# Retention layer before two MLPs, one core: chunk loads of 128 partitions and a two-round output

## The chip, the cores and the metric

The kernel runs on one core of one Trainium2 chip. The metric is the device time of the execution in microseconds (us), and the median of the runs is compared. A core has TensorE (PE, with its weight loads shown apart as PEld), VectorE (DVE), ScalarE (ACT), GpSimd (POOL) and SyncE (SP), which here only issues transfers. The engines run their own instruction streams in order and meet at semaphores.

## The reference

What is computed, cut to its core:

```python
# q, k, v: (2, 8, 576, 64)
scores = (q @ k^T) / sqrt(64)                       # per batch and head
ret = scores * where(i >= j, gamma[h] ** (i - j), 0)
attn = ret @ v
x = attn.transpose(0, 2, 1, 3).reshape(1152, 512)
# mixture of 4 experts, all of them for every token
p = domain_probs / (sum(domain_probs) + 1e-9)
for e in range(4):
    out += p[:, e:e+1] * (max(x @ w1[e], 0) @ w2[e])     # w1[e]: 512x1024, w2[e]: 1024x512
h = out @ w_in                                      # 512x2048
return (h * tanh(softplus(h))) @ w_out              # 2048x512
```

## The kernel before

The attention is computed in chunked form. A sequence of 576 tokens is cut into 9 chunks of 64 (`CH`, `CHUNKS`). For chunk t the output is the part inside the chunk (masked scores times v) plus the part of all earlier chunks, which is carried as a 64x64 matrix per head, the state, times q. Decay is applied to v ahead of time (`v_decay` on POOL) and to the rows of the output (`decayed` on DVE). There are two batches, and 64 rows are half of the 128 partitions, so the two batches lie in the two halves: `TOK[b]` is the half in which batch b has its tokens on the partitions, `FEAT[b]` the half in which it has its features.

**The loads.** A chunk of both batches is 1 MB. SP fetches it by `load_chunk(t)` in two transfers of 64 partitions by 8 KB (L403 and L404), into one of 4 slots (three in `qkv`, the fourth in `last_slot`). A slot has 5 columns: batch 0 has its v beside the q of batch 1, and so on, so that the two halves use different columns for the same kind of data, and each half of the transfer fills four of the five. From chunk 2 on SP first waits until chunk t-2 is there, and from chunk 4 on it also waits for the output of chunk t-4, which frees the slot. Before chunks 4 to 8 it issues two loads of 256 KB each for the MLP weights (`load_weights`, L413), of 128 partitions.

**A turn.** The program runs through `for t in range(CHUNKS)` on each engine. I call round t of it turn t.
PE does in turn t:
- scores of chunk t+1 and the state update of chunk t, interleaved (`scores_and_state`, L441 and L445, 64x64 matmuls). It waits for chunk t+1 to have landed, for the copy of the last state and for `v_decay(t)`.
- `output(t)` (L476): since state and v lie above each other in one column, and q and the masked scores in another, a single matmul of 128 rows does both terms at once. The first chunk has no state and goes by `first_output`, one batch after the other. Two PSUM banks take turns (`ps_o[t % 2]`).
- one or two of the eight first-layer tiles of the first token block (`plain_tile`, 12 matmuls each), placed by the tables `AHEAD` (before the output) and `BEHIND` (after it).

ACT copies the state out of PSUM in two halves (`state_copy`, L697), makes the rounded high part of the weights that have come (`job_hi`, L366) and of x (`first_hi`, L703), and applies relu to finished tiles (`plain_hi`, L714). DVE masks the scores, one instruction of 64 partitions for each batch (`masked`, L815), which writes them over q's place in the slot; it multiplies the output by its decay (`decayed`, L832, one instruction), makes row factors (`rows`, L823) and the low parts (`first_lo` L839, `plain_lo` L845). POOL decays v, one instruction of 64 partitions for each batch (L1026), and makes the low part of the weights (`job_lo`, L393).

**Weights.** All matmuls of the MLPs are done three times, as high by high, high by low and low by high part (L505 to L507). The table `IN_TURN` says in which turn which weight unit is split: "w1" and "w2" are units of the two layers, "s" is a job that forms sums of weight blocks (L380 to L388), since the later stages save multiplications by such sums. `FREE_UNITS` = 3 says how many units of w2 lie in memory that no chunk slot uses; the others wait until the chunks are through. The order on POOL at the end of the attention is unit 3 of w2, then the sums, then units 4 and 5.

After turn 8 PE does 36 matmuls of the second layer (`second(0, q)`, q 0 to 11, three units of tokens for each of the weight units 0 to 3), and then stage 2: `product` P1, two `second(1, q)`, P2, two more `second(1, q)`, then P6, which is the first to need the weight sums. `second(1, 0)` needs unit 4 of w2, `second(1, 3)` unit 5. `keep_warm` issues matmuls of zeros that only keep PE busy.

## Time and profile before

| | us |
|---|---|
| Median of 3 runs | 654.37 (653.7 to 657.46) |
| Profiled execution, its own time | 653.94 |
| Its span in the trace | 652.1 |
| Mean granted TensorE clock of that span | 0.975 |

| Engine | busy us | share of the span |
|---|---|---|
| PE (matmul) | 621.4 | 95% |
| PEld (weight load) | 554.8 | 85% |
| POOL | 288.7 | 44% |
| DVE | 244.4 | 37% |
| ACT | 235.1 | 36% |

Busy time is the union of an engine's instructions. Of the chain of work that ended last PE has 84% and transfers 9%. The trace gives every time from the span's start. PE's busy share by fortieths of the span (16.3 us each) is 60 to 90% in the first six and 90% or more in nearly all others, so what isn't PE at work lies in the first 96 us.

### The profile page before, as it was taken

How to read it: one execution, taken by the hardware profiler on the slowest of the kernel's cores; microseconds unless marked ns; L12 is line 12 of the kernel's file. 1: busy time of each engine (PE TensorE's matmuls, PEld its weight loads, DVE VectorE, ACT ScalarE, POOL GpSimd, SP SyncE). 2: the span in 40 equal slices, each digit the busy share in tenths (PEclk: the TensorE clock that was granted, in tenths of full speed). 3: DMA queues.
4: the chain of work that ended last, by engine and by line, in shares of the span. 5: the costliest groups of instructions: out<-in, count | busy, mean ns of one | idle time of the engine just before them, and what ended most of it. 6: DMA issues, size and time to landing. Idle time of an engine off the chain costs nothing.

```text
span 652.1 us, 9388 instructions
## 1 busy us (share of the span) xinstructions
PE 621.4 (95%) x3768; PEld 554.8 (85%) x3768; DVE 244.4 (37%) x370; ACT 235.1 (36%) x434; POOL 288.7 (44%) x239
## 2 busy tenths in 40 slices
PE   6677969999999999999999999999999999999997
PEld 3566859999999999989999989998979999989996
DVE  2457464333314333314333214334584333314324
ACT  1344242343223333222343223334554554334331
POOL 2356494554343554433544443542363544343300
PEclk8679889999999999999999999999999999999999
DMA  8998231232211133211233201231211233201004
GB/s 194 237 219 194 70 98 46 64 98 81 64 49 33 65 98 98 63 35 33 64 103 92 65 33 33 66 112 66 64 49 33 65 98 83 63 17 25 1 1 121
DMA packets 24170, 50.45 MB, mean 77 GB/s; under 512 B 3008, under 2 KB 3392, under 8 KB 22976
## 3 DMA queue, kind: packets, MB, share of 16 engines
q1 hardware_dynamic: 23152, 48.51, 27.8%
q10 hardware_dynamic: 976, 1.35, 0.8%
q8 instruction: 30, 0.49, 0.3%
q14 instruction: 12, 0.10, 0.1%
HBM read 47.49 MB, written 2.36 MB: 76 GB/s over the span
## 4 chain that ended last, share of the span: by engine, by line
PE 84%; DMA 9%; DVE 2%; POOL 2%; issue 1%; ACT 1%; SPq 1%; POOLq 0%
PE bank L506 28%; PE bank L507 28%; PE bank L505 28%; DMA qkv<-in_chunks 9%; POOL w_lo L393 1%; DVE xt L922 1%; PE bank L628 1%; SPq L403 0%; POOL ws L388 0%; SPq L413 0%; DVE acc_sb L892 0%; DVE acc_sb L896 0%; DVE h_lo L852 0%; DVE acc_sb L1004 0%; POOL ws_f L381 0%
## 5 line engine op out<-in xcount | busy, mean ns | idle before, releaser
L393 POOL TENSOR_TENSOR w_lo<-w_raw,w_hi 128x512 fp32r<-128x512 f32 x96 | 131.7, 1388 | 144.0 <-ACT w_hi L366 143.6
L505 PE MATMUL bank<-w_hi,h_hi 128*128 128x512 f32 x432 | 169.6, 393 | 5.0 <-POOL w_lo L393 5.0
L507 PE MATMUL bank<-w_hi,h_lo 128*128 128x512 f32 x432 | 170.3, 394 | 0.0
L506 PE MATMUL bank<-w_lo,h_hi 128*128 128x512 f32 x432 | 170.0, 394 | 0.0
L388 POOL TENSOR_TENSOR ws<-ws_f,ws 128x1024 fp32r<-128x1024 f32 x24 | 57.8, 2409 | 151.0 <-ACT ws L362 151.0
L879 DVE TENSOR_TENSOR h_act<-part,bank 128x384 f32<-128x384 f32 x96 | 52.9, 551 | 179.8 <-PE bank L507 179.8
L507 PEld LDWEIGHTS bank<-w_hi,h_lo 128*128 128x128 f32 x432 | 81.3, 188 | 17.6
L505 PEld LDWEIGHTS bank<-w_hi,h_hi 128*128 128x128 f32 x432 | 81.3, 188 | 14.9 <-POOL w_lo L393 5.3
L506 PEld LDWEIGHTS bank<-w_lo,h_hi 128*128 128x128 f32 x432 | 81.3, 188 | 9.8
L723 ACT ACTIVATE h_hi<-h_act 128x384 fp32r<-128x384 f32 x64 | 33.6, 526 | 108.1 <-DVE h_act L879 108.1
L505 PE MATMUL bank<-xa_hi,w_hi 128*128 128x384 f32 x192 | 67.2, 350 | 4.6 <-POOL w_lo L393 2.7
L507 PE MATMUL bank<-xa_hi,w_lo 128*128 128x384 f32 x192 | 66.2, 345 | 0.0
L506 PE MATMUL bank<-xa_lo,w_hi 128*128 128x384 f32 x192 | 66.0, 344 | 0.0
L733 ACT ACTIVATE part<-bank 128x384 f32<-128x384 f32 x72 | 35.2, 489 | 83.0 <-PE bank L507 82.2
L845 DVE SCALAR_TENSOR_TENSOR h_lo<-h_act,h_hi 128x384 fp32r<-128x384 f32 x64 | 46.1, 720 | 35.5 <-ACT h_hi L723 35.5
L852 DVE TENSOR_TENSOR h_lo<-h_act,h_hi 128x384 fp32r<-128x384 f32 x48 | 32.8, 683 | 69.2 <-ACT h_hi L728 69.1
L366 ACT ACTIVATE w_hi<-w_raw 128x512 fp32r<-128x512 f32 x96 | 56.8, 618 | 0.0
L505 PE MATMUL bank<-xt,ws 128*128 128x384 f32 x144 | 48.6, 338 | 1.2 <-DVE xt L922 1.2
L506 PE MATMUL bank<-xt,ws 128*128 128x384 f32 x144 | 48.6, 337 | 0.0
L507 PE MATMUL bank<-xt,ws 128*128 128x384 f32 x144 | 48.5, 337 | 0.0
L845 DVE SCALAR_TENSOR_TENSOR h_lo<-bank,h_hi 128x384 fp32r<-128x384 f32 x32 | 17.8, 557 | 81.3 <-ACT h_hi L714 81.3
L714 ACT ACTIVATE h_hi<-bank 128x384 fp32r<-128x384 f32 x32 | 15.7, 492 | 82.1 <-PE bank L507 82.1
(95 smaller groups left out, 895.8 us busy)
## 6 DMA issues: line engine op xcount, KB each, us to landing
w_raw<-in_weights SPq DMA_DIRECT2D x144, 256.0 KB, 2.8
qkv<-in_chunks SPq DMA_DIRECT2D x14, 512.0 KB, 10.1
last_slot<-in_chunks SPq DMA_DIRECT2D x4, 512.0 KB, 10.2
out<-acc_sb SPq DMA_DIRECT2D x6, 128.0 KB, 2.4
out<-acc_sb ACTq DMA_DIRECT2D x6, 128.0 KB, 2.9
out<-acc_sb SPq DMA_DIRECT2D x1, 384.0 KB, 3.9
out<-acc_sb ACTq DMA_DIRECT2D x1, 384.0 KB, 3.8
consts<-in_consts ACTq DMA_DIRECT2D x1, 146.0 KB, 5.1
```

Source lines behind the costliest of these rows:

```text
L366: act.activation(w_hi[:, int(kind == "w2"), x], w_raw[:, r % RAW], ACT.Copy).then_inc(s_wh, 1)
L388: pool.tensor_tensor(w_sum(x)[:, 1], ws_f[:, :], w_sum(x)[:, 0].bitcast(F32), ALU.subtract)\
L393: pool.tensor_tensor(w_lo[:, layer, x], w_raw[:, r % RAW], w_hi[:, layer, x].bitcast(F32), ALU.subtract).then_inc(s_wl, 1)
L505: pe.matmul(out, w[0], x[0], start=first, stop=False, **more)
L506: pe.matmul(out, w[0], x[1], start=False, stop=False, **more)
L507: return pe.matmul(out, w[1], x[0], start=False, stop=last, **more)
L714: act.activation(h_hi[:, tile_slot(s, i)], banks[6 + i % 2][:, 0:TC], ACT.Relu).then_inc(s_hh, 1)
L723: act.activation(h_hi[:, tile_slot(s, i)], h_act[:, i % 2], ACT.Relu).then_inc(s_hh, 1)
L733: act.activation(part[:, i], banks[6][:, 0:TC], ACT.Copy).then_inc(s_pt, 1)
L845: dve.scalar_tensor_tensor(h_lo[:, slot], full, 0.0, h_hi[:, slot].bitcast(F32), ALU.max, ALU.subtract).then_inc(s_hl, 1)
L852: dve.tensor_tensor(h_lo[:, slot], h_act[:, i % 2], h_hi[:, slot].bitcast(F32), ALU.subtract)\
L879: dve.tensor_tensor(h_act[:, i % 2], part[:, kept], banks[bank][:, 0:TC], op).then_inc(s_cc, 1)
```

## The change

It touches only the attention phase and the order of a few weight jobs around it.

- **Layout.** A slot has four columns of 128 partitions, one for each kind: v, k by tokens, k by features, q (`V, KTOK, KF, Q`). In each half stands the batch that belongs there. All four slots lie in `qkv`. A chunk is loaded by one transfer of 128 partitions by 8 KB.
- **Output in two rounds.** `output_of_state(t)` multiplies the state, which ACT now copies over the column KF, by q, 16 matmuls of 64x64; `output(t)` adds masked scores times v, again 16 of 64x64, onto the same PSUM. Each batch has one PSUM bank for all chunks, so the first round of chunk t waits for both `decayed` instructions of chunk t-1 (`s_xt`). Before, the banks alternated by chunk.
- **Masked scores** go to a tensor of their own (`masked_s`, two buffers) by one instruction of 128 partitions. `v_decay` is one instruction of 128 partitions too. `decayed` is two, one for each batch.
- **Weight order.** `FREE_UNITS` is 6. `EARLY_LOADS` puts 1, 2, 2, 2, 2, 2 and 1 weight loads behind (no longer before) the chunks 2 to 8. Unit 4 of w2 is split ahead of the sums, unit 5 after them. Tile 0 moves from behind the output of turn 3 to ahead of it, tiles 2 and 5 to behind the outputs of turns 4 and 6.
- **keep_warm** grows from 11 to 18 matmuls after the first 9.

```diff
-Y1, X0, X1, Z, Y0 = range(5)
-X, Y = (X0, X1), (Y0, Y1)
+V, KTOK, KF, Q = range(4)
...
-FREE_UNITS = 3
+FREE_UNITS = UNITS - 2
...
-AHEAD = {4: 1, 5: 2, 6: 4, 7: 5, 8: 7}
-BEHIND = {3: 0, 5: 3, 7: 6}
+AHEAD = {3: 0, 4: 1, 5: 3, 6: 4, 7: 6, 8: 7}
+BEHIND = {4: 2, 6: 5}
...
+EARLY_LOADS = ((0,), (1, 2), (3, 4), (5, 6), (7, 8), (9, 10), (11,))
...
-    for u in range(3):
-        add(IN_TURN, 6 + (u + 1) // 2, "w2", 0, u)
-    add(IN_TURN, 8, "w2", 0, 3)
-    add(IN_TURN, 8, "s", 0, 0)
-    for u in range(4, 6):
-        add(IN_TURN, 8, "w2", 0, u)
+    for u in range(5):
+        add(IN_TURN, 6 + (u + 2) // 3, "w2", 0, u)
+    add(IN_TURN, CHUNKS, "s", 0, 0)
+    add(IN_TURN, CHUNKS, "w2", 0, 5)
...
-                sp.dma_start(slot(t)[UPPER, 0:4], chunks_in[t, UPPER]).then_inc(s_slot[t % SLOTS], 16)
-                sp.dma_start(slot(t)[LOWER, 1:5], chunks_in[t, LOWER]).then_inc(s_slot[t % SLOTS], 16)
+                sp.dma_start(qkv[:, t % SLOTS], chunks_in[t]).then_inc(s_slot[t % SLOTS], 16)
...
-            for t in range(2, SLOTS):
+            for t in range(2, CHUNKS):
                 chunk_there(t - 2)
                 load_chunk(t)
-            for t in range(SLOTS, CHUNKS):
-                chunk_there(t - 2)
-                for r in range(2 * (t - SLOTS), 2 * (t - SLOTS) + 2):
+                for r in EARLY_LOADS[t - 2]:
                     load_weights(r)
-                load_chunk(t)
...
+            def output_of_state(t):
+
+                pe.wait_ge(s_st, BATCH * t)
+                pe.wait_ge(s_xt, BATCH * t)
+                for h in range(HEADS):
+                    x = h % 2
+                    for b in range(BATCH):
+                        mm = pe.matmul(ps_o[b][DH * x:DH * (x + 1), h // 2], part_of(t, FEAT[b], KF)[:, h],
+                                       part_of(t, FEAT[b], Q)[:, h], start=(h < 2), stop=False, skip_group_check=True)
+                mm.then_inc(s_qs, 1)
 
             def output(t):
 
-                pe.wait_ge(s_vd, BATCH * (t + 1))
-                pe.wait_ge(s_sm, BATCH * (t + 1))
-                pe.wait_ge(s_st, BATCH * t)
-                if t >= 2:
-                    pe.wait_ge(s_xt, t - 1)
-                for hp in range(PAIRS):
+                pe.wait_ge(s_vd, t + 1)
+                pe.wait_ge(s_sm, t + 1)
+                if t > 0:
+                    pe.wait_ge(s_qs, t)
+                for h in range(HEADS):
+                    x = h % 2
                     for b in range(BATCH):
-                        for x in range(2):
-                            mm = output_head(t, b, 2 * hp + x, slice(0, P))
+                        mm = pe.matmul(ps_o[b][DH * x:DH * (x + 1), h // 2], part_of(t, TOK[b], V)[:, h],
+                                       masked_s[TOK[b], t % 2, h], start=(t == 0 and h < 2), stop=True,
+                                       skip_group_check=True)
                 mm.then_inc(s_o, 1)
...
+                if t < PER_BLOCK:
+                    keep_warm(2)
+                if t > 0:
+                    output_of_state(t)
                 if t in AHEAD:
                     plain_tile(AHEAD[t])
-                if t == 0:
-                    keep_warm(3)
-                    first_output()
-                else:
-                    output(t)
+                output(t)
                 if t in BEHIND:
                     plain_tile(BEHIND[t])
+                if t < PER_BLOCK:
+                    keep_warm(2)
...
-                for b in range(BATCH):
-                    dve.tensor_tensor(part_of(t, TOK[b], Y[b]), ps_s[t % 2][FEAT[b]],
-                                      mask[FEAT[b]].unsqueeze(1).broadcast_to([CH, HEADS, CH]), ALU.mult).then_inc(s_sm, 1)
+                dve.tensor_tensor(masked_s[:, t % 2], ps_s[t % 2], mask.unsqueeze(1).broadcast_to([P, HEADS, CH]),
+                                  ALU.mult).then_inc(s_sm, 1)
...
-                dve.tensor_tensor(to.rearrange("p h (b c) -> p h b c", b=BATCH), ps_o[t % 2],
-                                  by.unsqueeze(2).broadcast_to([P, PAIRS, BATCH, CH]), ALU.mult).then_inc(s_xt, 1)
+                for b in range(BATCH):
+                    dve.tensor_tensor(to[:, :, CH * b:CH * (b + 1)], ps_o[b], by, ALU.mult).then_inc(s_xt, 1)
```

On SP, from chunk 2's load to chunk 5's (chunks are counted from 0). In this piece `qkv` and `last_slot` are the chunk slots, `w_raw` the weight ring. Before:

```order
L403 DMA qkv<-in_chunks 64x2048
L404 DMA qkv<-in_chunks 64x2048
L403 DMA last_slot<-in_chunks 64x2048
L404 DMA last_slot<-in_chunks 64x2048
L413 DMA w_raw<-in_weights 128x512 x2
L403 DMA qkv<-in_chunks 64x2048
L404 DMA qkv<-in_chunks 64x2048
L413 DMA w_raw<-in_weights 128x512 x2
L403 DMA qkv<-in_chunks 64x2048
L404 DMA qkv<-in_chunks 64x2048
```

After:

```order
L398 DMA qkv<-in_chunks 128x2048 x2
L407 DMA w_raw<-in_weights 128x512
L398 DMA qkv<-in_chunks 128x2048
L407 DMA w_raw<-in_weights 128x512 x2
L398 DMA qkv<-in_chunks 128x2048
L407 DMA w_raw<-in_weights 128x512 x2
L398 DMA qkv<-in_chunks 128x2048
```

Each chunk is one instruction in place of two, and the weights start earlier: chunk 4's load, the third row that is a chunk load in the piece after, has three weight loads ahead of it where it had two.

On POOL, from the last v decay to the weight sums (`qkv` is v being decayed, `w_lo` the split of a unit, `ws_f` and `ws` the sums). Before:

```order
L1026 TENSOR_TENSOR qkv<-qkv,consts 64x512 x2
L393 TENSOR_TENSOR w_lo<-w_raw,w_hi 128x512 x5
L380 TENSOR_TENSOR ws_f<-w_raw 128x256
L381 TENSOR_TENSOR ws_f<-w_raw 128x256
L383 TENSOR_TENSOR ws_f<-ws_f,w_raw 128x256
L385 TENSOR_TENSOR ws_f<-w_raw,ws_f 128x256
L388 TENSOR_TENSOR ws<-ws_f,ws 128x1024
L393 TENSOR_TENSOR w_lo<-w_raw,w_hi 128x512 x4
```

After:

```order
L1009 TENSOR_TENSOR qkv<-qkv,consts 128x512
L388 TENSOR_TENSOR w_lo<-w_raw,w_hi 128x512 x6
L375 TENSOR_TENSOR ws_f<-w_raw 128x256
L376 TENSOR_TENSOR ws_f<-w_raw 128x256
L378 TENSOR_TENSOR ws_f<-ws_f,w_raw 128x256
L380 TENSOR_TENSOR ws_f<-w_raw,ws_f 128x256
L383 TENSOR_TENSOR ws<-ws_f,ws 128x1024
L388 TENSOR_TENSOR w_lo<-w_raw,w_hi 128x512 x3
```

One more unit of w2 is split ahead of the sums, and one fewer behind them.

## Rows read from the trace of the kernel before

**Rows 1.** Chain of waits, 0 to 62 us: start us, us, what
```profile
1.39 7.45 DMA qkv<-in_chunks
...
32.91 13.64 DMA qkv<-in_chunks
...
47.94 13.73 DMA qkv<-in_chunks
```

**Rows 2.** Busy time by stretch: stretch, its length, engines, granted clock, DMA share, GB/s
```profile
14.00:18.86 4.86, 3.21 (x99) 2.32 (x99) 2.07 (x3) 1.81 (x3) 2.08 (x2) 1.00 1.02 216
31.54:38.76 7.22, 6.04 (x108) 5.42 (x108) 3.40 (x5) 3.35 (x6) 3.35 (x3) 0.76 1.04 228
...
23.00:24.50 1.50, 1.38 (x23) 1.19 (x23) 0.05 (x2) 0.00 (x0) 0.00 (x0) 0.50 1.14 365
29.50:31.00 1.50, 0.00 (x0) 0.00 (x0) 0.69 (x1) 0.63 (x1) 0.00 (x0) 1.00 1.13 350
...
96.00:652.00 556.00, 550.52 (x2761) 496.28 (x2759) 193.95 (x305) 202.33 (x378) 237.53 (x196) 1.00 0.21 61
```

**Rows 3.** Timeline of PE, turns 0 to 5: start, us, instruction [idle before <-releaser]
```profile
15.87 1.43 PE L476 MATMUL bank<-qkv 64*64 64x64 f32 x32
...
31.57 0.27 PE L441 MATMUL bank<-qkv 64*64 64x64 f32 x2 [2.94 <-DMA qkv<-in_chunks]
...
42.36 0.44 PE L505 MATMUL bank<-xa_hi,w_hi 128*128 128x384 f32 x1 [2.41 <-POOL w_lo L393]
...
46.15 1.16 PE L476 MATMUL bank<-qkv 128*64 128x64 f32 x32
47.24 0.27 PE L441 MATMUL bank<-qkv 64*64 64x64 f32 x2
...
48.33 0.44 PE L505 MATMUL bank<-xa_hi,w_hi 128*128 128x384 f32 x1
...
50.62 1.15 PE L476 MATMUL bank<-qkv 128*64 128x64 f32 x32
51.70 0.44 PE L505 MATMUL bank<-xa_hi,w_hi 128*128 128x384 f32 x1
```

**Rows 4.** Timeline of PE, turn 7 to stage 2
```profile
64.82 0.66 PE L505 MATMUL bank<-xa_hi,w_hi 128*128 128x384 f32 x1 [1.94 <-issue]
...
76.00 0.50 PE L505 MATMUL bank<-w_hi,h_hi 128*128 128x512 f32 x1
...
84.29 0.33 PE L505 MATMUL bank<-xb_hi,w_hi 128*128 128x384 f32 x1
...
90.47 0.71 PE L505 MATMUL bank<-w_hi,h_hi 128*128 128x512 f32 x1 [4.95 <-POOL w_lo L393]
...
95.96 0.34 PE L505 MATMUL bank<-xt,ws 128*128 128x384 f32 x1
```

**Rows 5.** Timeline of POOL, 38 to 97 us
```profile
38.81 2.15 POOL L1026 TENSOR_TENSOR qkv<-qkv,consts 64x512 f32<-64x512 f32 x2 [3.65 <-DMA qkv<-in_chunks]
...
56.48 2.53 POOL L393 TENSOR_TENSOR w_lo<-w_raw,w_hi 128x512 fp32r<-128x512 f32 x2
...
79.76 1.46 POOL L380 TENSOR_TENSOR ws_f<-w_raw 128x256 f32<-128x256 f32 x1
...
86.11 2.36 POOL L388 TENSOR_TENSOR ws<-ws_f,ws 128x1024 fp32r<-128x1024 f32 x1 [1.23 <-ACT ws L362]
88.43 7.86 POOL L393 TENSOR_TENSOR w_lo<-w_raw,w_hi 128x512 fp32r<-128x512 f32 x4
```

**Rows 6.** Timeline of ACT, turn 5
```profile
50.73 0.49 ACT L714 ACTIVATE h_hi<-bank 128x384 fp32r<-128x384 f32 x1 [0.70 <-PE bank L507]
51.11 1.14 ACT L366 ACTIVATE w_hi<-w_raw 128x512 fp32r<-128x512 f32 x2
```

**Rows 7.** Timeline of DVE, 52 to 60 us
```profile
52.04 0.55 DVE L845 SCALAR_TENSOR_TENSOR h_lo<-bank,h_hi 128x384 fp32r<-128x384 f32 x1
...
59.49 0.41 DVE L823 TENSOR_TENSOR part<-consts 128x256 f32<-128x256 f32 x1
```

More of the change, by code:

```diff
@@ L183, in build @@
         sb("w_ahead", [P, UNITS + FREE_UNITS, DM], stack=ahead)
-        last_slot = sb("last_slot", [P, 5, HEADS, CH], stack=ahead)
+        masked_s = sb("masked_s", [P, 2, HEADS, CH], stack=ahead)
         ahead.close()
@@ L241, in build @@
         ps_state = banks[2][:, :].rearrange("p (h c) -> p h c", h=HEADS)
-        ps_o = [banks[3 + i][:, :].rearrange("p (h b c) -> p h b c", h=PAIRS, b=BATCH) for i in range(2)]
+        ps_o = [banks[3 + b][:, 0:PAIRS * CH].rearrange("p (h c) -> p h c", h=PAIRS) for b in range(BATCH)]
         s_slot = [sem(f"s_slot{i}") for i in range(SLOTS)]
@@ L440, in scores_head @@
             def scores_head(t, b, h):
-                return pe.matmul(ps_s[t % 2][FEAT[b], h], part_of(t, FEAT[b], X[b])[:, h],
-                                 part_of(t, FEAT[b], Y[b])[:, h], start=True, stop=True)
+                return pe.matmul(ps_s[t % 2][TOK[b], h], part_of(t, FEAT[b], KF)[:, h], part_of(t, FEAT[b], Q)[:, h],
+                                 start=True, stop=True)
             def state_head(t, b, h):
-                return pe.matmul(ps_state[FEAT[b], h], part_of(t, TOK[b], Z)[:, h], part_of(t, TOK[b], X[b])[:, h],
+                return pe.matmul(ps_state[TOK[b], h], part_of(t, TOK[b], KTOK)[:, h], part_of(t, TOK[b], V)[:, h],
                                  start=(t == 0 and h == 0), stop=True, skip_group_check=True)
@@ L639, in _ @@
             scores(0)
-            keep_warm(8)
+            keep_warm(6)
             for t in range(CHUNKS):
@@ L696, in state_copy @@
                 for b in range(BATCH):
[L697 removed]
+                    act.activation(part_of(t + 1, FEAT[b], KF), ps_state[TOK[b]], ACT.Copy).then_inc(s_st, 1)
             def first_hi(t):
[L701 removed]
+                act.wait_ge(s_xt, BATCH * (t + 1))
                 full, hi, lo = x_chunk(t)
@@ L753, in _ @@
                     plain_hi(*divmod(AHEAD[t], ITEMS))
-                if t + 1 < CHUNKS:
-                    for job in IN_TURN.get(t, ()):
-                        job_hi(act, job)
+                for job in IN_TURN.get(t, ()):
+                    job_hi(act, job)
                 first_hi(t)
@@ L759, in _ @@
                     plain_hi(*divmod(BEHIND[t], ITEMS))
-            for job in IN_TURN[CHUNKS - 1]:
+            for job in IN_TURN[CHUNKS]:
                 job_hi(act, job)
@@ L813, in masked @@
                 dve.wait_ge(s_sc, t + 1)
-                for b in range(BATCH):
-                    dve.tensor_tensor(part_of(t, TOK[b], Y[b]), ps_s[t % 2][FEAT[b]],
-                                      mask[FEAT[b]].unsqueeze(1).broadcast_to([CH, HEADS, CH]), ALU.mult).then_inc(s_sm, 1)
+                dve.tensor_tensor(masked_s[:, t % 2], ps_s[t % 2], mask.unsqueeze(1).broadcast_to([P, HEADS, CH]),
+                                  ALU.mult).then_inc(s_sm, 1)
             def rows(i):
@@ L1074, in chunks @@
         vt, kt, kf, qf = by_tokens(v), by_tokens(k), by_features(k), by_features(q)
-        upper = np.stack([qf[1], vt[0], kf[1], kt[0]], axis=2)
-        lower = np.stack([kf[0], vt[1], kt[1], qf[0]], axis=2)
+        upper = np.stack([vt[0], kt[0], kf[1], qf[1]], axis=2)
+        lower = np.stack([vt[1], kt[1], kf[0], qf[0]], axis=2)
         return np.concatenate([upper, lower], axis=1)
```

47 lines of the change are left out of this document (13 added, 34 removed).

## The prediction

> **What bounds the kernel now.** I read the page's busy shares first: PE works through nearly all of the span after the first 96 us, 550.5 of 556 us busy at full clock [rows 2]. Nothing in the change touches that part, so I cost only the stretch up to PE's first matmul with weight sums (P6), which starts at 95.96 us [rows 4], and carry the rest over. Within the stretch I read the chain of waits next. Its long pieces are chunk transfers: 7.45 us for the first, over 13 us for the later ones [rows 1]. Then the windows: while chunks move, the DMA share is 1.02 to 1.04 and the rate 216 to 228 GB/s [rows 2]. The transfers never pause and set the pace, and PE waits for each chunk, 2.94 us for chunk 4 at 31.57 [rows 3]. The last chunk lands at 47.94 + 13.73 = 61.7 us [rows 1]. After it PE has its own backlog, reaches the second layer at 76.00, and then sits 4.95 us at 90.47 for a `w_lo` that stands behind the weight sums on POOL [rows 4, 5]. So there are two things to win: the transfer rate, and that wait.
>
> **The rate.** A chunk is 1.05 MB, and at 216 GB/s it takes 4.9 us. There are two windows in which two weight loads of 128 partitions go through between the chunk halves, and the same queue then moves 365 and 350 GB/s [rows 2], at a DMA share only a tenth higher. The engines are as busy in both, so a load of 64 partitions uses them at lower yield. A chunk loaded on 128 partitions has the weights' shape with longer rows, so I take the lower of the two, 350. The bounds are 216 (nothing gained) and 365.
>
> The Trainium skill ("SBUF — State Buffer", section on the DMA port swizzle) says the same of the halves: partitions 0 to 63 reach only 8 of 16 ports, and 1 MiB moved at 196 GB/s there against 328 on 128 partitions. This case's trace has 216 and 350. By 328 the chunk time below would be 3.2 us in place of 3.0, and the end 1.2 us later.
>
> **When chunk 4 is there.** The first chunk lands at 8.84 [rows 1]; 4.9 of that is transfer, so 3.9 is issue and completion, which stay. Ahead of the end of chunk 4 stand five chunks (5.24 MB), three weight loads (0.79) and some 0.23 MB of constants: 6.26 MB, 17.9 us at 350. Chunk 4 lands at 21.8, against 31.5. Up to there PE has no say: a turn without tiles is one scores round of 1.1 us (47.24 to 48.33 [rows 3]), two output rounds and four `keep_warm`, about 3 us, as long as one chunk.
>
> **PE from turn 3 to the second layer.** From turn 3 on, chunk and weights together need 1.57 MB, 4.5 us each, and PE needs as much or more, so PE takes over. Its work: five scores-and-state rounds of 1.1; eight tiles of 2.3 (48.33 to 50.62 [rows 3]); and six outputs. An output was 1.1 us (50.62 to 51.70 [rows 3]) for 32 records of 128 rows. Now it is 64 records of 64 rows. Two rows bound this: the scores-and-state round does 64 such records in 1.1 us, with four quarters of the array in turn, while `first_output` needed 1.43 us for 32 [rows 3], with consecutive matmuls in the same rows of the array. The new rounds alternate the two batches and so the row halves, like the first, so I take 1.1, no change. Sum: 5.5 + 18.4 + 6.6 = 30.5 us.
>
> The Trainium skill ("TensorE: Matmul & The Clock Gate", Part 3, "The mechanism") speaks against splitting a matmul of 128 rows in two unless they overlap, and lets a weight load overlap a running matmul only where the row group differs. The code alternates them, and the rows above agree. Were they not to overlap, it is the second rival below.
>
> **New stalls, worked out from rows.**
> - Turn 3: tile 0 now stands ahead of the output and needs its `w_lo`. POOL must first decay v of chunk 4: 2.15 us for two instructions of 64 partitions before [rows 5], one now, 1.1 to 1.3 since the same columns pass once. With a `w_lo` of 1.27 (2.53 for two [rows 5]) that is 2.5 us after landing. PE's scores and state output cover 1.7. Stall 0.8.
> - Turn 4: `job_hi` for tile 1 stands on ACT behind tile 0's relu: 0.5 + 0.6 [rows 6], then 1.3 on POOL, with hand-overs 2.9 us from tile to tile. PE has 2.2 us of rounds. Stall 0.6.
> - The added wait: `output_of_state(t)` waits for `decayed(t-1)`, and behind it on PE are the tile and the output, on which in turn all engines wait. `decayed` runs behind `plain_lo` on DVE. After a tile: relu 0.5 [rows 6], low part 0.55, two `decayed` of 0.4 (a 128x256 took 0.41) [rows 7] and hand-overs give 2.1 us, against 1.65 of output and scores round on PE. Some 0.2 to 0.4 in turns 4 and 6; nothing in 5 and 7, behind a second tile; in turn 8, where there is no scores round to cover it, 1.7. Together 2.3.
>
> The masking becomes one instruction in place of two, which helps DVE but isn't on this path. T, the start of the second layer, is 21.8 + 30.5 + 0.8 + 0.6 + 2.3 = 56.0.
>
> **Clock and gaps.** The trace of before is no clean sum either. After PE's 2.94 and 2.41 us waits the granted clock fell to 0.50, which is the 1.2 GHz level, and a tile took 3.8 us (42.36 to 46.15 [rows 3]) in place of 2.3; and there was a 1.94 us gap that nothing in the profile explains [rows 4]. I allow one such tile (1.5) and one such gap (1.9): T = 59.4, against 76.00. That saves 16.6 us. The `keep_warm` added in turns 0 to 2 lies in time that belongs to the transfers; if these are faster than 350, it costs up to 7 x 0.23 us (a matmul of 512 columns, a third of a `second` in the tail below).
>
> **The tail.** From 76.00 to 95.96 are 20.0 us [rows 4]. 4.95 is the wait. The stretch from 90.47 took 5.5 for four `second` of 0.69 ((84.29 - 76.00)/12 [rows 4]) and one product of 1.1, that is 3.8 of work; 1.7 was low clock after the wait. Now unit 4 is split ahead of the sums. Unit 5 is needed at T + 8.3 + 1.1 + 1.4 + 1.1 + 0.7 = T + 12.6. On POOL: unit 4 done at T + 2.1 (relu, `job_hi`, `w_lo` after the last tile, which ends 0.6 before T); the sums took 8.7 us from the first at 79.76 to the end of `ws` at 88.47, ACT's copy among it [rows 5], and give T + 10.8; unit 5 takes 1.3 to 2.0 (7.86/4 [rows 5]) and is there at T + 12.2 to 12.8. So the wait shrinks to 0 to 0.5; I take 0.5. Saved: 4.95 + 1.7 - 0.5 = 6.1.
>
> **Sum.** 16.6 + 6.1 = 22.7 us. The profiled execution took 653.94 by its own time, 0.4 below the median of the runs; 653.94 - 22.7 = 631.2. **I predict 631.**
>
> **Rivals.**
> - The rate stays near 216, because the engines and not the partitions limit it (for: share 1.02 at 216; against: 350 at 1.13). Ahead of chunk 8's end are 12.5 MB: 58 + 3.9 = 62 us. Then a scores round, two tiles, two outputs and the stall of turn 8 are 9.5, T = 71.5, and with the low clock of such a pace 73 to 74. With the tail 2 to 3 + 6.1 saved: 645. Chance 0.10.
> - The rate comes, but the 64x64 rounds don't overlap. Twelve rounds of 1.4 in place of 0.55 from turn 3: +10, 641. Chance 0.12.
> - Slower: the PE of the new turns, with short waits in each, never leaves the 1.2 GHz level from turn 3 to P6. Tiles show the price, 3.8 against 2.3, a factor of 1.65. On 30.5 + 13.3 us of work that is +28.5, less the 1.5 allowed: 658. It decides only if the low level holds in all six turns and the second layer; before, waits of 2 to 3 us brought it on, and it went back each time while PE worked. Chance 0.04.
> - The change doesn't do what it says: chunk 8's load stands on SP behind weight loads that wait for `w_lo` of units 1 and 2 and for the output of turn 4. Both come at about 29 to 31 us, chunk 8 lands by 40, and PE wants it at 45. There are 5 us of cover, so this costs nothing unless turn 4 is 5 us late; then each further us is one us. It is in the range, with no chance of its own.
>
> **How the numbers follow.** Forecast 0.74, rivals 0.10, 0.12, 0.04. The forecast's own range: without allowance for clock and gaps and without the turn 8 stall 626, with the rate of 365 and shorter hand-overs 623; with two more low-clock tiles or a second gap 635. The range takes in the second rival: 622 to 642. What a measurement of this kernel can tell from no change is about 0.5%, 3.3 us. Faster by more than that: the forecast, the first two rivals, less what I may have overlooked in each: 0.92. Same 0.03, slower 0.05.
>
> **What would show it.** Chunk loads land at about 5 us in place of 10; window rates of 330 or more between chunks; chunk 4's scores at 22 us; tiles ahead of outputs at 2.3 us with the clock at 1.00; each output round at 0.6; second layer at 56 to 60; no wait over 1 us before P6; P6 at 73. Wrong would be: rates of 220 (first rival), output rounds of 1.4 (second), clock 0.50 past 35 us (third), PE waiting for chunk 8 (fourth), or any change in the 556 us after P6, which I hold fixed.

## The result, and the profile after

The changed kernel takes 636.98 us (median of 4 runs, 635.42 to 638.36) beside 654.04 for the kernel before in the same set (652.5 to 657.46): a ratio of 0.973, with a 95% interval of 0.968 to 0.978. That is 17.1 us less; I had said 631, 6 us below what came. Two later sets of runs gave 634.3 and 634.65 for the same kernel (ratios 0.974 and 0.972), so 17 to 18 us is its gain. The profiled execution took 638.36, with a span of 636.58, 15.6 less than before (652.14).

From the page of the changed kernel come its busy times, the rates in GB/s by fortieths of the span (15.9 us each), and the group of chunk loads (KB each, us from issue to landing):

```profile
PE 617.0 (97%) x4031; PEld 548.8 (86%) x4031; DVE 238.1 (37%) x370; ACT 234.9 (37%) x434; POOL 278.9 (44%) x230
...
GB/s 344 285 205 116 85 50 66 96 71 66 67 33 67 92 75 67 67 33 67 84 82 67 67 33 68 82 84 34 67 33 34 67 114 84 67 0 26 2 0 124
...
qkv<-in_chunks SPq DMA_DIRECT2D x9, 1024.0 KB, 5.7
```

The chain of waits and the windows answer [rows 1] and [rows 2] (columns as there):

```profile
0.74 5.47 DMA qkv<-in_chunks
```

```profile
6.20:9.30 3.10, 3.04 (x35) 2.22 (x36) 2.59 (x7) 0.00 (x0) 1.04 (x1) 1.00 1.03 433
9.30:12.80 3.50, 3.50 (x103) 2.06 (x102) 2.72 (x5) 1.11 (x2) 2.00 (x2) 1.00 1.02 417
12.80:18.80 6.00, 3.71 (x133) 2.49 (x132) 1.98 (x4) 1.89 (x4) 1.59 (x2) 1.00 0.99 389
...
81.10:636.00 554.90, 549.82 (x2748) 495.59 (x2748) 193.76 (x305) 201.68 (x376) 235.67 (x193) 1.00 0.20 61
```

One chunk transfer is left in the chain where there were many. The DMA share is still about 1, but it now stands for 389 to 433 GB/s instead of 216 to 228. PE's busy share of the long part at the end is what it was.

The timeline of PE through turns 1 to 4 answers [rows 3] (L472 is the new `output_of_state`, L485 the new `output`, L432 and L436 scores and state, L492 the first of a product's three matmuls):

```profile
17.23 0.58 PE L472 MATMUL bank<-qkv 64*64 64x64 f32 x24 [2.11 <-issue]
17.99 0.69 PE L485 MATMUL bank<-masked_s,qkv 64*64 64x64 f32 x32 [0.18 <-PE bank L472]
...
21.96 0.69 PE L472 MATMUL bank<-qkv 64*64 64x64 f32 x30 [0.86 <-issue]
...
23.98 0.27 PE L432 MATMUL bank<-qkv 64*64 64x64 f32 x2
...
27.16 0.27 PE L436 MATMUL bank<-qkv 64*64 64x64 f32 x2 [2.02 <-issue]
...
27.91 0.45 PE L492 MATMUL bank<-xa_hi,w_hi 128*128 128x384 f32 x1
...
30.22 0.69 PE L485 MATMUL bank<-masked_s,qkv 64*64 64x64 f32 x32
...
33.68 0.37 PE L432 MATMUL bank<-qkv 64*64 64x64 f32 x2 [2.07 <-issue]
```

After the first chunk no wait of PE in this execution names a transfer. What is left is four gaps with no releaser (the rows say `<-issue`), 7.06 us together (before: 3.93 us in three). Both output rounds last 0.6 to 0.7, and the first tile 2.3.

The turns' end and the tail, which answer [rows 4]: the wait of turn 8, the start of the second layer (T), P6, and P7, the product behind P6.

```profile
58.74 0.69 PE L472 MATMUL bank<-qkv 64*64 64x64 f32 x32 [1.30 <-DVE xf L820]
...
62.28 0.50 PE L492 MATMUL bank<-w_hi,h_hi 128*128 128x512 f32 x1
...
75.77 0.34 PE L492 MATMUL bank<-xt,ws 128*128 128x384 f32 x1
...
81.10 0.44 PE L492 MATMUL bank<-xt,ws 128*128 128x384 f32 x1 [2.73 <-ACT part L723]
```

The 4.95 us wait for `w_lo` is gone, and a wait of 2.73 stands in a place that had none. Followed back, it comes from DVE. First DVE, with four low parts of the inputs for the product with weight sums (L909, function `t_lo`) and behind them the `h_act` that P7 needs; then the two steps of ACT between:

```profile
71.74 2.02 DVE L909 TENSOR_TENSOR xt<-xs_a,xt 128x768 fp32r<-128x768 f32 x1 [1.64 <-ACT xt L737]
...
77.62 2.03 DVE L909 TENSOR_TENSOR xt<-xs_b,xt 128x768 fp32r<-128x768 f32 x1
79.58 0.54 DVE L866 TENSOR_TENSOR h_act<-part,bank 128x384 f32<-128x384 f32 x1
```

```profile
80.15 0.52 ACT L713 ACTIVATE h_hi<-h_act 128x384 fp32r<-128x384 f32 x1 [4.90 <-DVE h_act L866]
80.58 0.47 ACT L723 ACTIVATE part<-bank 128x384 f32<-128x384 f32 x1
```

After this wait PE is at the 1.2 GHz level for a time, and so spends longer on the same work (windows behind P7; 0.50 and 0.78 are the granted clock):

```profile
82.00:84.00 2.00, 2.00 (x7) 1.81 (x6) 0.00 (x0) 0.85 (x2) 0.74 (x1) 0.50 0.00 0
84.00:86.00 2.00, 2.00 (x9) 1.74 (x9) 0.00 (x0) 0.58 (x1) 1.28 (x1) 0.78 0.00 0
```

**The span's difference in three pieces.** Up to T: 76.00 - 62.28 = 13.7 saved. T to P6: 19.96 before, 13.49 after, 6.5 saved. P6 to the end: 556.2 before, 560.8 after, 4.6 lost. Sum 15.6. In the first piece the clock counts as well: from 6 us to T the mean granted clock was 0.80 before and is 0.97 now.

### The profile page after: what moved, and what is told of

It is laid out like the page before. It is cut to its first block, busy times and chain, and to the rows that moved or that the text cites. A ratio compares the mean times of both kernels' runs of the same rounds, so it can differ in the third digit from the quotient of the medians.

```text
span 636.6 us, 9885 instructions
## 1 busy us (share of the span) xinstructions
PE 617.0 (97%) x4031; PEld 548.8 (86%) x4031; DVE 238.1 (37%) x370; ACT 234.9 (37%) x434; POOL 278.9 (44%) x230
## 4 chain that ended last, share of the span: by engine, by line
PE 90%; DVE 4%; issue 2%; POOL 2%; ACT 1%; DMA 1%; DVEq 0%; ACTq 0%; POOLq 0%
PE bank L492 29%; PE bank L493 29%; PE bank L494 29%; DVE xt L909 2%; PE bank L432 1%; DMA qkv<-in_chunks 1%; PE bank L622 1%; POOL w_lo L388 1%; PE bank L472 1%; PE bank L485 1%; PE bank L615 1%; PE bank L436 0%; DVE acc_sb L879 0%; DVE acc_sb L883 0%; DVE h_lo L839 0%
## 5 line engine op out<-in xcount | busy, mean ns | idle before, releaser
L388 POOL TENSOR_TENSOR w_lo<-w_raw,w_hi 128x512 fp32r<-128x512 f32 x96 | 129.6, 1366 | 153.7 <-ACT w_hi L361 153.7
L492 PE MATMUL bank<-w_hi,h_hi 128*128 128x512 f32 x432 | 169.6, 393 | 0.0
L383 POOL TENSOR_TENSOR ws<-ws_f,ws 128x1024 fp32r<-128x1024 f32 x24 | 57.9, 2414 | 152.2 <-ACT ws L357 152.2
L494 PEld LDWEIGHTS bank<-w_hi,h_lo 128*128 128x128 f32 x432 | 81.3, 188 | 17.6
L492 PEld LDWEIGHTS bank<-w_hi,h_hi 128*128 128x128 f32 x432 | 81.4, 188 | 10.0 <-POOL w_lo L388 0.4
L492 PE MATMUL bank<-xa_hi,w_hi 128*128 128x384 f32 x192 | 66.2, 345 | 0.0
L492 PE MATMUL bank<-xt,ws 128*128 128x384 f32 x144 | 48.9, 340 | 4.0 <-ACT part L723 2.7
```

The source lines that it names most:

```text
L383: pool.tensor_tensor(w_sum(x)[:, 1], ws_f[:, :], w_sum(x)[:, 0].bitcast(F32), ALU.subtract)\
L388: pool.tensor_tensor(w_lo[:, layer, x], w_raw[:, r % RAW], w_hi[:, layer, x].bitcast(F32), ALU.subtract).then_inc(s_wl, 1)
L492: pe.matmul(out, w[0], x[0], start=first, stop=False, **more)
L494: return pe.matmul(out, w[1], x[0], start=False, stop=last, **more)
```

## The experiments

T and the sum of the gaps without a releaser ahead of it are read from each run's PE timeline. In most traces single records of `keep_warm` are missing and leave holes of 0.16 to 0.33 us, which are not counted as gaps. The kernel after and those made from it stand first; times are in us:

| Kernel | median us | ratio to before | gaps, us | T | P7 - T | end - P7 |
|---|---|---|---|---|---|---|
| changed, first set | 636.98 | 0.973 | 7.1 | 62.28 | 18.8 | 555.5 |
| changed, again | 634.3 | 0.974 | 3.9 | 57.93 | 18.8 | 555.4 |
| changed, third time | 634.65 | 0.972 | 5.2 | 60.75 | 18.8 | 553.8 |
| transfers in halves | 659.89 | 1.012 | 13.2 | 81.94 | 18.8 | 556.3 |
| in four quarters | 638.8 | 0.980 | 5.2 | 62.08 | 18.8 | 556.1 |
| one chunk in flight | 637.56 | 0.979 | 4.8 | 63.96 | 18.8 | 555.4 |
| sums first | 632.58 | 0.970 | 6.3 | 59.00 | 18.2 | 553.9 |
| `t_lo` moved | 632.89 | 0.973 | 4.6 | 60.04 | 16.9 | 553.9 |
| `decayed` first | 633.89 | 0.973 | 5.5 | 61.14 | 18.5 | 554.0 |
| three edits together | 632.46 | 0.970 | 4.4 | 58.08 | 17.0 | 553.9 |
| fewer `keep_warm` | 635.73 | 0.975 | 6.7 | 58.24 | 18.8 | 555.2 |
| before, wide load | 635.16 | 0.974 | 3.4 | 57.63 | 22.3 | 553.7 |
| the same, with edits for the tail | 633.4 | 0.971 | 4.7 | 59.01 | 19.8 | 553.8 |
| before | 654.04 | 1 | 3.9 | 76.00 | 22.4 | 553.8 |

### What the width of the load does

**The change with the transfer in halves.** All else is the changed kernel.

```diff
-sp.dma_start(qkv[:, t % SLOTS], chunks_in[t]).then_inc(s_slot[t % SLOTS], 16)
+sp.dma_start(qkv[UPPER, t % SLOTS], chunks_in[t, UPPER]).then_inc(s_slot[t % SLOTS], 16)
+sp.dma_start(qkv[LOWER, t % SLOTS], chunks_in[t, LOWER]).then_inc(s_slot[t % SLOTS], 16)
```

> The changed kernel, with each chunk loaded in two transfers of 64 partitions again; nothing else differs. Theory, the width of the load sets the rate: windows between chunks show some 216 GB/s in place of 390 to 430, the last chunk lands at about 62 us, PE waits 2 us or more for most chunks, and the time is 643 to 650. Rival, the gain came from the weight order and the shorter turns: the time stays within 2 us of 637.

It took 659.89 (658.87 to 660.93), ratio 1.012 (1.006 to 1.017): the whole gain is gone and 7 us more. Windows and two of the gaps of PE:

```profile
9.30:12.80 3.50, 3.38 (x36) 2.37 (x37) 0.69 (x1) 0.00 (x0) 1.04 (x1) 1.00 1.00 213
12.80:18.80 6.00, 3.50 (x102) 1.91 (x101) 1.44 (x3) 1.82 (x3) 1.04 (x1) 1.00 1.01 224
```

```profile
33.52 1.12 PE L473 MATMUL bank<-qkv 64*64 64x64 f32 x30 [3.39 <-issue]
...
41.68 0.37 PE L437 MATMUL bank<-qkv 64*64 64x64 f32 x2 [3.68 <-issue]
```

The rate is that of before, 213 and 224 GB/s, at a DMA share of 1.00. The same bytes go into the same places; in the same stretches of the changed kernel it is 417 and 389. What differs is the width, and two transfers instead of one; the four transfers below tell these apart. The Trainium skill ("SBUF — State Buffer", "Door 1: The DMA port swizzle") gives asymptotes of 218 GB/s for partitions 0 to 63 and 436 for all 128; the rows are near both.

The last chunk lands at 63.51, as expected, but the rest went otherwise. PE waits for only three chunks (4.09, 0.84 and 2.16 us) and not for most. Its time goes into gaps without a releaser, 13.2 us here, nearly twice those of the changed kernel and 9.3 more than before the change, and into low clock, with a mean granted clock of 0.84 from 6 us to T (before: 0.80). T is later than before by 5.9, and the time lies 10 us above the 643 to 650 of my theory. What makes the gaps so long here is shown below.

**The kernel before with a wide load.** The old layout of five columns and the old output in one round, but a single transfer of 128 partitions by 10 KB, a fifth of it zeros.

```diff
-sp.dma_start(slot(t)[UPPER, 0:4], chunks_in[t, UPPER]).then_inc(s_slot[t % SLOTS], 16)
-sp.dma_start(slot(t)[LOWER, 1:5], chunks_in[t, LOWER]).then_inc(s_slot[t % SLOTS], 16)
+sp.dma_start(slot(t)[:, 0:5], chunks_in[t]).then_inc(s_slot[t % SLOTS], 16)
```

> The kernel before, whose chunk is loaded in one transfer of 128 partitions by five columns (10 KB, of which 2 KB are zeros); output in one round, order of the weights and all the rest as before. Theory, the wide load is the main part: last chunk by 42 us, second layer at about 60 in place of 76, the wait for w_lo behind the sums still there, time 638 to 643. If the two rounds and their extra PE instructions cost something, turns 1 to 4 have fewer gaps without a releaser than in the changed kernel. Rival, the width alone does little because the old order of PE, POOL and DVE work binds: above 648.

635.16 (634.78 to 636.99), ratio 0.974 (0.969 to 0.979), below the 638 to 643 that I expected and as good as the changed kernel, though each chunk is 1.31 MB. Its wait in the tail is still there:

```profile
72.09 0.79 PE L504 MATMUL bank<-w_hi,h_hi 128*128 128x512 f32 x1 [4.94 <-POOL w_lo L393]
```

So the wide transfer alone brings everything up to T (57.63), and with it as much in the median as the whole change, though its tail is the old one. The two-round output brings nothing by itself; it is what lets one transfer of four columns do without the zeros.

**Four transfers of 2 KB rows**, one for each column, still 128 partitions wide:

```diff
-sp.dma_start(qkv[:, t % SLOTS], chunks_in[t]).then_inc(s_slot[t % SLOTS], 16)
+for c in range(4):
+    sp.dma_start(qkv[:, t % SLOTS, c], chunks_in[t, :, c]).then_inc(s_slot[t % SLOTS], 16)
```

> The changed kernel, with each chunk loaded in four transfers of 128 partitions by one column (rows of 2 KB in place of 8 KB), the same bytes. The gaps without a releaser on PE come every 128 matmul records, with one 16 KB packet of the instruction queue in each. Theory A (a fetch of instructions waits behind large packets of the same DMA engine): the gaps of 2.0 to 2.1 us shrink below 1 us, time 3 to 6 us less. Theory B (it waits for its share of a busy engine whatever the packet size, or takes a fixed time): gaps as they were, time within 2 us.

638.8 (637.4 to 641.27), ratio 0.980 (0.973 to 0.986). In the stretches of the windows above the rates are 295 and 334 GB/s in place of 417 and 389: the start is slower, but T is 62.08, inside the spread of the changed kernel. Against the 634.3 to 637 of that kernel a cost of 2 to 4 us is likely but not separated. So four transfers, with rows of 2 KB, cost some rate, and still move 38 and 49% more than two transfers of half the width in the same stretches: the loss in the halves is one of width and not of the number of transfers. Theory A on the gaps fell: they are 5.2 us, one of them 3.06.

**One load in flight at a time** (SP waits for the chunk before, not the one before that):

```diff
-                chunk_there(t - 2)
+                chunk_there(t - 1)
```

> The changed kernel, but SP issues a chunk load only when the chunk before has landed, so that one is in flight in place of two and the DMA engines have pauses. Theory A (an instruction fetch is slow because it shares DMA engines with the loads): the gaps without a releaser in turns 1 to 4, 7 us together in the changed kernel's profile, fall below 3 us; chunks come later, one each 4 to 5 us, so the time is 634 to 640. Theory B (a fetch takes its time whatever else moves): gaps of the same 7 us, and the time 638 to 642.

637.56 (635.28 to 639.97), ratio 0.979 (0.975 to 0.984), where the changed kernel in the same set had 634.3. The gaps were 4.8 us, no fewer than the 3.9 of that run and not below the 3 of theory A, and the waits for chunks came back (1.18, 0.93 and 1.92 us). From its chain of waits, one chunk:

```profile
13.76 4.81 DMA qkv<-in_chunks
```

That is 1.05 MB in 4.81 us from issue to landing, 218 GB/s for the chunk. A weight load issued before it was still under way until 15.78. This issue leaves a hole in the transfers: from 13.76 to 14.50 the engines move 42 GB/s, from 14.5 to 16 they move 183, and only then 410. So two chunks in flight are worth about 3 us, and a thinner queue doesn't take the gaps away.

### What stands between the chunks and P7

**The weight sums ahead of unit 4**, as in the kernel before:

```diff
-    for u in range(5):
+    for u in range(4):
...
+    add(IN_TURN, CHUNKS, "w2", 0, 4)
```

> The changed kernel, with the weight sums split ahead of unit 4 of w2, as before the change. Theory A (the tail is now bound by DVE's four low parts of the x sums, which start after the sums' copy): PE waits about 2 us for unit 4, but the wait of 2.7 us before P7 shrinks by as much; time within 1.5 us of the changed kernel. Theory B (the order is worth what the old wait was, as I predicted): 4 to 5 us slower.

632.58 (632.17 to 634.17), ratio 0.970 (0.965 to 0.975). P7 stands at T + 18.2 with a wait of 2.46, against T + 18.8 and 2.73. PE doesn't wait for unit 4 or 5. The early split of unit 4, to which I had given the 4.95 us, is not needed for it. POOL's rows, with T at 59.00:

```profile
54.66 3.95 POOL L389 TENSOR_TENSOR w_lo<-w_raw,w_hi 128x512 fp32r<-128x512 f32 x3 [4.20 <-ACT w_hi L362]
58.57 0.74 POOL L376 TENSOR_TENSOR ws_f<-w_raw 128x256 f32<-128x256 f32 x1
...
65.64 3.99 POOL L389 TENSOR_TENSOR w_lo<-w_raw,w_hi 128x512 fp32r<-128x512 f32 x2
```

The first row holds the units 1 to 3, all ahead of T. Before the change unit 3 was split 1.9 us behind T (77.93), and the sums started 3.8 behind it (79.76 [rows 5]). Here they start 0.4 ahead of it, and unit 4, the first of the pair at 65.64, is done before PE wants it at T + 9.4. That unit 3 comes early fits `FREE_UNITS` = 6, since this unit no longer waits for the outputs that free the slots; no run changes `FREE_UNITS` alone. The clock has a part in this run's time too: it was 1.00 throughout (mean of the profiled execution), 0.993 to 0.996 in those of the changed kernel.

**One `t_lo` moved.** Of the four low parts ahead of P7's inputs on DVE one is put behind them:

```diff
-            for n in range(4):
+            for n in range(3):
...
+                        if s == 2 and i == C11:
+                            t_lo(0, 3)
```

> The changed kernel, with DVE's fourth low part of the x sums moved behind its first addition of partial products. Theory (the 2.7 us wait before P7 is that chain: four low parts of 2.0 us, addition, relu, the copy of P6's result): the wait shrinks to 0.7 or less, time 2 to 3 us less than the changed kernel beside it, since the clock doesn't fall after it either. Rival (P7's wait is ACT's own queue): no change.

PE's wait before P7, and DVE ahead of it:

```profile
76.92 0.45 PE L492 MATMUL bank<-xt,ws 128*128 128x384 f32 x1 [0.82 <-ACT part L723]
```

```profile
73.42 2.05 DVE L909 TENSOR_TENSOR xt<-xs_a,xt 128x768 fp32r<-128x768 f32 x1
75.39 0.54 DVE L866 TENSOR_TENSOR h_act<-part,bank 128x384 f32<-128x384 f32 x1
```

P7 comes at T + 16.9 instead of 18.8: moving 2.03 us of DVE work off the path moved PE by 1.94 us, and no low clock follows (553.9 from P7 to the end). That DVE holds P7 is shown. The time was 632.89 (631.63 to 634.85), 1.4 below the changed kernel of the same set (633.24 to 634.77). The ranges overlap, so the size of the gain in the median is not settled.

**`decayed` ahead of the low part of a tile on DVE**, for the wait that the change adds:

```diff
+                decayed(t)
...
-                decayed(t)
```

> The changed kernel, with DVE's two decayed instructions ahead of the low part of the tile (plain_lo of AHEAD) in turns 3 to 8. Theory (the state output waits for decayed, which waits behind plain_lo): the 1.30 us wait of turn 8 becomes 0.7 to 0.9 and the short one of turn 6 goes; 0.5 to 1 us less in all. Rival (a low part that comes later holds up tiles or the second layer): equal or slower by up to 1 us.

The wait of turn 8 fell from 1.30 to 1.04, less than the 0.7 to 0.9 of my theory, and 633.89 against 634.3 is no difference. The low part ahead of `decayed` is thus 0.26 of this wait. That the rest is the chain through `decayed` itself is my reading, and no run tests it.

**All three together.** 

> The changed kernel with three edits of order: the weight sums ahead of unit 4 of w2, one low part on DVE behind the work that P7 waits for, and the two decayed instructions ahead of the low part of a tile. Theory: each frees only what the trace showed waiting, and these do not add up in full. P7 comes 16.5 to 17.2 us after the start of the second layer in place of 18.8, the turn 8 wait is 1.0 in place of 1.3, in all 2 us: 630 to 633. Rival (the DVE chain is not what holds P7, the next late thing takes its place): P7 at 18.2 or more after the start of the second layer, time as the changed kernel's in the same call, within 0.7 us.

P7 at T + 17.0, the turn 8 wait 1.04. The median was 632.46 (630.57 to 635.79), ratio 0.970 (0.966 to 0.974), beside 634.65 and 0.972 (0.969 to 0.976) for the changed kernel. That is the lowest median of all and 2.2 us below the changed kernel, as the pieces say, but the intervals overlap.

**The wide load of before with two edits meant for the tail.** 

> The kernel of before with the wide load of five columns (one-round output, two banks by turns), and now also with both edits of the tail: unit 4 of w2 is split ahead of the weight sums, and one of the four low parts of the last tile group on DVE stands behind the work that the product before P7 needs. Theory (the transfers are one gain, the tail is a second and separate one, and the two-round output brings nothing by itself): second layer from 57 to 60 us as in the run with five columns, the 4.94 us wait for w_lo gone, P7 about 17 us after the start of the second layer, so 628 to 632, below the changed kernel by 3 to 8 us. Rival (the two-round output does bring something, because the one-round output has its own stalls on the masked scores): second layer not before 60, and a time no better than the changed kernel's, 634 to 638.

The edit of the weight order doesn't do what this text says:

```diff
-    add(IN_TURN, 8, "s", 0, 0)
+    add(IN_TURN, CHUNKS, "s", 0, 0)
     for u in range(4, 6):
-        add(IN_TURN, 8, "w2", 0, u)
+        add(IN_TURN, CHUNKS, "w2", 0, u)
```

The sums still stand ahead of unit 4. What the edit changes is that ACT makes the high part of unit 3 ahead of its work on the last output (`first_hi`) instead of behind it. It took 633.4 (631.51 to 634.9), ratio 0.971 (0.967 to 0.974), above the 628 to 632 of my theory. PE in the tail, and POOL from unit 3 on:

```profile
70.91 0.50 PE L504 MATMUL bank<-w_hi,h_hi 128*128 128x512 f32 x1 [2.38 <-POOL w_lo L393]
```

```profile
59.12 1.29 POOL L393 TENSOR_TENSOR w_lo<-w_raw,w_hi 128x512 fp32r<-128x512 f32 x1 [2.91 <-ACT w_hi L366]
60.38 0.74 POOL L380 TENSOR_TENSOR ws_f<-w_raw 128x256 f32<-128x256 f32 x1
...
68.87 7.14 POOL L393 TENSOR_TENSOR w_lo<-w_raw,w_hi 128x512 fp32r<-128x512 f32 x4
```

The unit at 59.12 is unit 3, and unit 4 is the first of the four at 68.87. Half of the `w_lo` wait stayed, 2.38 of 4.94, because unit 4 still stands behind the sums; the other half went because the sums start at T + 1.4 instead of T + 3.8. So the start of the sums sets this wait, here as in the run with the sums first. Whether unit 4 ahead of the sums would end it with five columns too, and with it what the memory that four columns leave is worth, stays open. P7 came at T + 19.8 and not 17, behind that wait. T is 59.01, as expected: the one-round output with the wide load reaches it once more as early as the changed kernel.

### The gaps, and keep_warm

**Without the 12 `keep_warm` matmuls of turns 0 to 2:**

```diff
-                if t < PER_BLOCK:
-                    keep_warm(2)
```

> The changed kernel without the 12 keep_warm matmuls of turns 0 to 2 (two ahead of and two behind the output in each). Theory A (they only fill waits for the transfers): the second layer starts within 1 us of where it did, the granted clock in turns 1 to 3 falls no more than before, time within 2 us of the changed kernel's in the same call. Theory B (they keep the clock up): granted clock 0.50 in at least one of the turns 1 to 3 and 1.5 to 4 us more. The same run tells something of the gaps that no releaser explains: if they belong to the count of PE instructions, they stay at the same counts of matmul records as in the changed kernel (222 to 226, 346 to 354, and so on in steps of about 128) and so come some 12 records later in the program; if they belong to a place in the program (a turn, a kind of round), they stay at the place and come 12 records earlier in the count.

**The changed kernel again, twice.** 

> The changed kernel as it is, beside the three others of this call, as their yardstick: its runs lay at 635.5 and 638.3 so far. If gaps without a releaser are what scatters, their places (every 128 matmul records from record 226 on) are the same as in its first profile and their lengths are not.

 

> The changed kernel once more, the yardstick of this set of runs. Expected: 634 to 638 us; gaps without a releaser of 4 to 7 us in all ahead of the second layer, at the same counts of matmul records, in steps of about 128.

635.73 (634.1 to 638.81) without them beside 634.65 (633.45 to 635.22): no difference that these runs can tell. The granted clock dips in the same region, 0.75 and 0.82 of full speed in 20 to 24 and 24 to 28 us without them, 0.90 and 0.67 in 24 to 28 and 28 to 32 us with them. That these matmuls cost time or hold the clock is not to be seen here.

The gaps are more telling. First the run without the 12 matmuls, then the changed kernel of the same set (both PE):

```profile
15.72 0.56 PE L472 MATMUL bank<-qkv 64*64 64x64 f32 x18 [2.33 <-issue]
...
21.64 0.64 PE L472 MATMUL bank<-qkv 64*64 64x64 f32 x20 [3.05 <-issue]
```

```profile
17.34 0.58 PE L472 MATMUL bank<-qkv 64*64 64x64 f32 x24 [2.08 <-issue]
...
21.54 0.69 PE L472 MATMUL bank<-qkv 64*64 64x64 f32 x30 [0.31 <-issue]
```

A round of `output_of_state` has 32 matmuls. With 6 `keep_warm` fewer ahead of it the first gap stands in front of its last 18 instead of its last 24; with 10 fewer, the second in front of its last 20 instead of 30. Counted from the program's start the gaps are ahead of matmul records 221, 347, 599 and 850 in the one and 219, 343 and 468 in the other, in the profiled run of the first set at 221, 347, 473 and 599. The second trace lacks two records of `keep_warm` ahead of the first gap, four ahead of the second and five ahead of the third, which makes them 221, 347 and 473 too. So the gaps belong to the count of PE's instructions, in steps of 126 matmuls or a multiple of it, and to no place in the program. And around each, or just ahead of it, there is one packet of the instruction queue. Here are the four half microseconds from 14.5, 19.5, 24.5 and 31.0 us of the changed kernel, with the gaps 15.12 to 17.23, 21.10 to 21.96, 25.14 to 27.16 and 31.6 to 33.68 (packets, MB, share of the 16 engines' time):

```profile
q8 instruction: 1, 0.02, 13.7%
```

```profile
q8 instruction: 1, 0.02, 13.8%
```

```profile
q8 instruction: 1, 0.02, 15.2%
```

```profile
q8 instruction: 1, 0.02, 12.1%
```

The page's total is 32 such packets, 0.52 MB together and 16 KB each, and PE has 4031 matmuls and as many weight loads: 252 instructions for a packet, 126 matmuls, which is the step of the gaps. The share gives how long a packet took: 13.7% of 16 engines' 0.5 us is 1.1 us. The trace has their starts as well, 14.81, 19.61, 24.62 and 31.38, and so their ends, 15.90, 20.71, 25.84 and 32.34. PE goes on at 17.23, 21.96, 27.16 and 33.68, that is 1.33, 1.25, 1.32 and 1.34 us behind them, even in the second case, where the packet had ended before the gap began. All 14 profiled runs together have 53 such gaps, and each ends 1.2 to 1.7 us behind the end of the packet whose turn it is by the count. Where a step of 126 has no gap, PE got there no sooner than that. So PE goes on only when the packet is there, and this is shown by timing in every run, though none moved a packet by itself.

The traces show too why the gaps grow. The next packet starts some time after PE has begun on the instructions of the last one: in the changed kernel 2.2 to 4.2 us after it for the first four, while chunks and weights were moving, and 1.1 us at 45.75, where the DMA share was 0.01. In the run with halves it is 4.8 to 6.9 us for the first five, and 1.1 at 70.03, when the chunks were through. Before the change it was 4.6 to 6.3, but there PE had fewer instructions in a turn and waited for chunks besides. So the packets of instructions come later while data is moving, and PE stands still where its matmuls are so short that 126 of them take less time than the next packet needs to come. From one restart to the next it was 4.7 to 6.5 us here; in the later stages a packet lasts some 25 us (packets at 64.2, 90.7 and 115.6), and no trace has a gap there.

## Why the prediction was right, and where it was wrong

**The rate: right, and too low.** I took 350 GB/s with 365 as the upper bound; it was 389 to 433. Both weight loads of [rows 2] stood between slow transfers, so their windows may have held some of these as well. The first rival (216) fell, and the halves show that it would have cost more than the 645 I gave it.

**Chunk 4: the data early, PE late.** I had it land at 21.8 and PE begin its scores then. It landed at 20.02, but PE began only at 23.98. The step that failed is "Up to there PE has no say": the new turns 1 and 2 put more records in the same time, and two gaps of 2.11 and 0.86 fell into them.

**Turns 3 to 8: right as a sum, on wrong terms.** From 23.98 to T are 38.3 us; I had 30.5 of work, 3.7 of stalls and 3.4 allowed, 37.6. The rounds and tiles were as I had them, and the second rival (rounds that don't overlap) fell by the 0.69 of both outputs. The stalls were about 1.6 and not 3.7: 1.30 in turn 8 where I had 1.7, 0.25 in turn 6; those of turns 3 and 4 hardly showed. The one tile at low clock was there, from 35.17 to 38.32, 3.15 us in place of 2.3, less than the 3.8 I had taken. But the gaps were 4.1 in these turns where I allowed 1.9. I took them as chance, while they are part of the program: PE has 140 matmul records a turn now, 108 before, so a packet more in every four turns, and no waits for chunks under which they could hide. Stalls that were too dear paid for gaps that were too cheap, so the sum is partly luck.

**T is a spread, not a number.** I predicted 59.4. The changed kernel's three profiled runs have 62.28, 57.93 and 60.75, a mean of 60.3; with the five runs that differ from it only in an order or in 12 matmuls of `keep_warm` it is 59.7. So the 16.6 us saved there were right to about one us on average. Within the three the gaps make most of the difference: without them T would be 55.2, 54.0 and 55.5. The low clock doesn't tell them apart, since the mean granted clock from 6 us to T is 0.97 in all three. In the run with the sums first it is 1.00, and T is 59.00 in spite of 6.3 us of gaps.

**The tail: right to P6, wrong behind it.** I had 6.1 saved and so P6 at 13.9 us behind T; measured 6.5 and 13.5. POOL's path came nearly as I had it: the sums were done at T + 10.7 (10.8 forecast), and the last bit of waiting, for unit 5, was 0.44 on PE's weight loads, where I had 0.5. But the wait for unit 4 would have gone without its early split too, as the run with the sums first shows; I had not seen that unit 3 comes earlier as well and the sums with it. The step that failed is the first one of all, "Nothing in the change touches that part". The price is 4.6 us of the 556: 2.9 between P6 and P7 (5.33 us, before 2.41), then about 1.7 at the 1.2 GHz level. DVE in the kernel before, the first of the four `t_lo` and the `h_act` behind them, and then PE's P7:

```profile
87.84 1.44 DVE L922 TENSOR_TENSOR xt<-xs_a,xt 128x768 fp32r<-128x768 f32 x1 [4.38 <-ACT xt L747]
...
95.05 0.54 DVE L879 TENSOR_TENSOR h_act<-part,bank 128x384 f32<-128x384 f32 x1
```

```profile
98.37 0.34 PE L505 MATMUL bank<-xt,ws 128*128 128x384 f32 x1
```

They ran under the 4.95 us wait and the slow clock behind it [rows 4], and were done when P7 wanted them, at 98.37. I asked what was late next only for PE's wait at `w_lo`, and followed POOL and not DVE, which waits for the same sums. In three sets of runs the changed kernel had 2.7 to 2.8 us there; the low clock came in two of the three.

**The other rivals.** The clock did not stay at 1.2 GHz (0.993 in the mean). Chunk 8's load was issued at 39.12 and nothing waited for it, as I had said.

**The sum.** 16.6 + 6.1 = 22.7 forecast. Measured in the profiled run 13.7 + 6.5 - 4.6 = 15.6; with a T of 60.3 it would be 17.6, and the medians of the three sets say 17.1, 17.8 and 18.0. So of the miss of 5 us the larger and lasting part, 2.9 us and with the low clock 4.6, is the DVE chain; T came 0.9 later than forecast in the mean, and 2.9 in the profiled run, by the gaps. That the number came within 1% owes something to luck inside the sum up to T, and nothing in it allowed for the DVE chain.

## What to carry to other kernels

Make a transfer as wide as the partitions before anything else: in this kernel that one line was worth all the gain up to T, even with a fifth of the bytes wasted, and in the median as much as the whole change (635.16 us against 634.3 to 637). When a wait is removed, list every engine that was waiting for the same thing and what it did in that time; the next one late was DVE, 5 us further on, in the part that I had declared fixed. And where a timeline shows gaps that nothing explains, count instructions from one to the next and look for the instruction packets before taking them as chance: a change that issues more and smaller instructions while data is moving meets them more often.

## What the runs showed of the hardware

- Gaps of PE of 0.2 to 3.7 us at steps of 126 matmuls, each ending 1.2 to 1.7 us behind the end of one 16 KB packet of the instruction queue, and only after chunks or weights had been moving. Their sum ahead of T was 3.9 to 7.1 us in three executions of the same kernel, and this makes most of the spread of its T, 57.9 to 62.3.
- Loads of 128 partitions moved 389 to 433 GB/s, those of 64 partitions 213 to 228, both at a DMA share of about 1.
- Decaying v by one instruction of 128 partitions takes 1.04 us in six of nine chunks and up to 1.5 in the others, about as much as each of the two of 64 partitions before (2.15 for both [rows 5]).
- POOL and DVE slow each other. The first of these is of the changed kernel, where DVE was subtracting 128x768 tensors at the same time; the second of the run with the sums first, where the same instruction ran without that:

```profile
65.00 1.46 POOL L376 TENSOR_TENSOR ws_f<-w_raw 128x256 f32<-128x256 f32 x1
```

```profile
59.27 0.74 POOL L377 TENSOR_TENSOR ws_f<-w_raw 128x256 f32<-128x256 f32 x1
```

The Trainium skill ("SBUF — State Buffer", "Who interferes with whom") says that a DVE instruction with two inputs in SBUF contends with a GpSimd instruction that reads it. The trace agrees: 1.46 against 0.74 us, twice as long. It goes the other way as well: DVE's `xs_b<-xf`, a 128x768 subtraction with both inputs in SBUF, took 1.50 us beside POOL in the changed kernel (65.77) and 0.95 in the run with the sums first (62.48), where POOL stood still until 62.98.
